# Identity products across a hand-over, and weight splits placed ahead of the folds

## The chip, the cores and the metric

The kernel runs on one core of a Trainium2 chip. The metric is the device time of one execution in microseconds (us); lower is better. A core has TensorE (PE in the profile, with its weight loads as PEld), VectorE (DVE), ScalarE (ACT), GpSimd (POOL) and SyncE (SP), which run their own instruction streams and meet on semaphores, and DMA queues that SP, ACT and POOL feed.

## The reference, cut to what matters

Four batches of 576 tokens, 512 features. Attention that keeps the top 32 scores of each row; a layer that sends each token to one of 8 experts; then a Fourier mixing layer with a two-layer network. All is float32.

```python
def _moe_ref(x, w_gate, w_local, w1, w2):          # experts
    ...
            h = np.maximum(x[b, s] @ w1[e], 0.0)
            out[b, s] = p[e] * (h @ w2[e])

def _moe2_ref(x, w_ch1, w_ch2):                    # mixer
    X = np.fft.fft(x, axis=1)
    X = np.fft.fft(X, axis=2)
    mixed = np.real(X).astype(np.float32)
    u = x + mixed
    mu = np.mean(u, axis=-1, keepdims=True)
    var = np.mean((u - mu) ** 2, axis=-1, keepdims=True)
    un = (u - mu) / np.sqrt(var + 1e-06)
    ch = np.maximum(un @ w_ch1, 0.0) @ w_ch2
    return (u + ch).astype(np.float32)
```

## The kernel before, in words

The program is a row of blocks: attention, routing, experts, mixer. In a block each engine has its own stream; at the end of a block all engines meet, and none starts the next block before the last has come.

**Early blocks.** Seven blocks of 128 tokens (NA = 7) go through their expert while attention and routing still run. Their hidden values and results live in the two buffers `stage[0]` and `stage[1]` (the `h`, `xT` and `y` of `early_buffers`). The last early result is scattered to the arrays `y_d` and `r_d` by POOL at the head of the experts' block (`early_scatter`, L264), and each of its two transfers adds to the semaphore `s_yo` of the early part. So far only POOL waits for that semaphore, at the very end of the experts' block.

**experts (L1080 on).** Fifteen blocks of 128 tokens. For each, PE multiplies the gathered tokens by `w1` (`hidden`, L1195: 32 float32 products of 128 columns, two records in the trace for each), turns the next block's tokens (L1183) and multiplies the hidden values by `w2`, split into a high and a low part (`output`, L1208 to L1210). ACT makes the high part (L1236), DVE the low part (L1252). SP's stream `load` decides block by block whether new weights have to be loaded: when the expert is the one already there it only raises the weight semaphore (L1167), otherwise it issues the DMA and that raises it. PE's `hidden` and ACT's split of `w2` wait for these semaphores, of the first block too. POOL gathers tokens (L1277) and scatters results (L1293).

**mixer (L1306 on).** For each batch: `fold` on DVE (L1715 to L1722) makes even and odd parts of the rows that SP (`xa`) and ACT (`xb`) have loaded; PE's `sequence` (L1478, five groups of three products) transforms along the tokens, ACT copies each group out (`u_out`, L1580), PE's `channels` (L1492, L1495) transforms along the features, ACT copies (`p_out`, L1589), DVE adds and takes moments (`low_high`, `add_a`, `moments`), ACT takes the square root (`spread`, L1596), DVE normalises (L1763), PE turns the tiles (`turn`, L1505), ACT copies them out (L1611). The network then runs in passes: PE's `hidden` and `output` (L1462 to L1464), with the following batch's transforms put in between. The network's weights come in 16 chunks of 512 KB through the two `stage` buffers; `split_w` on ACT (L1617) makes the high part of a chunk, `split_w` on DVE (L1768) the low part, and the load of chunk c (`load_w`, L1402) waits until chunk c - 2 has been split. All orders are written out by hand: an engine does its steps in the order of the code, so a step that waits holds back all that stands behind it.

In the mixer before, ACT does the first four `split_w` between `u_out` and `p_out`, and DVE does its first two behind the folds of the first batch and the other two behind those of the second.

Of the kernel before, what the change touches and what calls it, by code (L numbers as in the profile page):

```python
# [13 lines left out]
ACT = mybir.ActivationFunctionType  # L14
# [8 lines left out]
P = 128  # L23
# [13 lines left out]
NA = 7  # L37
# [1042 lines left out]
def experts(nc, env):  # L1080
# [5 lines left out]
    with ExitStack() as ctx:  # L1086
# [21 lines left out]
        ps_x = pb("ps_bx", [P, NC, P])  # L1108
# [12 lines left out]
        def used_blocks(eng):  # L1121
            return eng.value_load(env["blk_e"][0:1, NBLK + 2:NBLK + 3], min_val=0, max_val=NBLK)

        def blocks(eng, used, body):

            with eng.Fori(0, (SURE - 2) // 2) as i:
                for c in range(2):
                    body(i, c)
            for j in range((SURE - 2) // 2 * 2, SURE):
                body(j // 2, j % 2)  # L1130

            def rest(j):
                if j < NBLK:
                    with eng.If(used > j):
                        body(j // 2, j % 2)
                        rest(j + 1)

            rest(SURE)
# [12 lines left out]
        @block.sync  # L1151
        def _(sp):
            def expert(j):
                at = bass.ds(j + 2, 1) if not isinstance(j, int) else slice(j + 2, j + 3)
                return sp.value_load(env["blk_e"][0:1, at], min_val=0, max_val=E - 1)

            def load(i, c):
                j = 2 * i + c
                e, before = expert(j), expert(j - 2)

                def renew(load_w, s):

                    wait_apart(sp, s[c], 16 * i + 16, s_sp)
                    with sp.If(e != before):
                        load_w(sp, env, e, (NA + c) % 2, s[c])
                    with sp.Else():
                        sp.sem_inc(s[c], 16)  # L1167

                wait_apart(sp, s_h1, 2 * j + 2, s_sp)
                renew(load_w1, s_w1)  # L1170
                wait_apart(sp, s_w2lo, NQ * j + NQ, s_sp)
                renew(load_w2, s_w2)

            blocks(sp, used_blocks(sp), load)

        @block.tensor
        def _(pe):
            def turn(i, c, n):

                pe.wait_ge(s_x[c], 16 * (i + n // 2) + 16)  # L1180
                pe.wait_ge(s_xT, 2 * i + n + 1)
                for k in range(NC):
                    mm = pe.transpose(ps_x[:, k, :], x[c][:, k * P:(k + 1) * P], ident[:, :])  # L1183
                mm.then_inc(s_t, 1)

            def hidden(i, c):
                j = 2 * i + c
                pe.wait_ge(s_w1[c], 16 * i + 32)
                pe.wait_ge(s_xT, j + 2)
                for half in range(2):  # L1190
                    pe.wait_ge(s_hlo, 2 * j + half + 1)
                    for m in range(NF // 2):
                        f0 = (half * NF // 2 + m) * P
                        for k in range(NC):
                            mm = pe.matmul(ps_h[half][:, m, :], w1[c][:, k, f0:f0 + P], xT[c][:, k, :],  # L1195
                                           start=(k == 0), stop=(k == NC - 1))
                    mm.then_inc(s_h1, 1)

            def output(i, c):
                j = 2 * i + c  # L1200
                pe.wait_ge(s_yv, j + 1)
                for m in range(NF):
                    if m % (NF // 2) == 0:
                        pe.wait_ge(s_hlo, 2 * j + m // (NF // 2) + 3)
                    if m % (NF // NQ) == 0:
                        pe.wait_ge(s_w2lo, NQ * j + m // (NF // NQ) + 1 + 2 * NQ)
                    first, last = m == 0, m == NF - 1
                    pe.matmul(ps_y[c][:, :], h_hi[c][:, m, :], w2_hi[:, m, :], start=first, stop=False)  # L1208
                    pe.matmul(ps_y[c][:, :], h_hi[c][:, m, :], w2_lo[:, m, :], start=False, stop=False)
                    mm = pe.matmul(ps_y[c][:, :], h_lo[c][:, m, :], w2_hi[:, m, :], start=False, stop=last)  # L1210
                mm.then_inc(s_y, 1)

            for s, n in ((s_t, 2), (s_h1, 4), (s_y, 2)):
                pe.sem_inc(s, n)
            turn(0, 0, 0)
            used = used_blocks(pe)

            def body(i, c):
                hidden(i, c)
                if_used(pe, used, i, c + 1, lambda: turn(i, 1 - c, c + 1))  # L1220
                output(i, c)

            blocks(pe, used, body)

        @block.scalar
        def _(act):
# [81 lines left out]
def mixer(nc, env, w_ch, out):  # L1308
# [9 lines left out]
    NU = 5  # L1318
# [6 lines left out]
    with ExitStack() as ctx:  # L1325
        def sb(name, shape, dt=F32):
            return ctx.enter_context(nc.sbuf_tensor(name, shape, dt))
# [12 lines left out]
        p_sb = [sb(f"p_sb{n}", [P, HC + 1]) for n in range(2)]  # L1340
        lo = [sb(f"lo{n}", [P, HC + 1]) for n in range(2)]
        hi = [sb(f"hi{n}", [P, HC + 1]) for n in range(2)]
        stats = [sb(f"stats{w}", [P, 6]) for w in range(2)]
        mv = [[sb(f"mv{n}_{w}", [P, 2]) for w in range(2)] for n in range(2)]
        sd = [[sb(f"sd{n}_{w}", [P, 1]) for w in range(2)] for n in range(2)]
# [35 lines left out]
        def _(sp):  # L1381
            def load_a(n):
                r0, rows = rows_of(n)
                sp.dma_start(xa[n % RING][0:rows, :], env["y_d"][r0:r0 + rows, :]).then_inc(s_in[n % RING], 16)
# [12 lines left out]
                    load_b(n)  # L1397

            def load_w(c):
                if c >= 2:  # L1400
                    sp.wait_ge(s_wlo, c - 1)
                sp.dma_start(stage[c % 2][:, :], w_ch[c, :, :]).then_inc(s_stage[c % 2], 16)  # L1402

            def store_a(n):
# [16 lines left out]
                    r0 = (G * g + n) * P  # L1421
                    sp.dma_start(u[n][:, :], src[r0:r0 + P, :]).then_inc(s_ul[n], 16)

            for n in range(3):
                load_a(n)
            for c in range(2):
                load_w(c)
            for n in range(3, 6):
                load_a(n)
            for c in range(2, 6):  # L1430
                load_w(c)
# [28 lines left out]
        def _(pe):  # L1460
            def three(out_, hi1, lo1, hi2, lo2, first, last):
                pe.matmul(out_, hi1, hi2, start=first, stop=False)  # L1462
                pe.matmul(out_, hi1, lo2, start=False, stop=False)  # L1463
                return pe.matmul(out_, lo1, hi2, start=False, stop=last)  # L1464

            def sequence(b, m):

                part, tab = (ee, env["c_seq"]) if m < 3 else (oo, env["s_seq"])
                c0 = P * m if m < 3 else P * (m - 3)
                w = 1 if m == 2 else P  # L1470
                if m < 2:
                    pe.wait_ge(s_te, 6 * b)
                else:
                    pe.wait_ge(s_us, NU * b + m - 1)
                for k in range(3):
                    if m == 0:
                        pe.wait_ge(s_fold, 3 * b + k + 1)
                    mm = pe.matmul((ps_u, ps_t)[m % 2][0:w, 0:N1], part[b % 2][k][0:ROWS[k], c0:c0 + w],  # L1478
                                   tab[0:ROWS[k], k, :], start=(k == 0), stop=(k == 2))
                mm.then_inc(s_u, 1)  # L1480
# [70 lines left out]
                mm.then_inc(s_y, 1)  # L1551

            pe.wait_ge(env["s_tab"], 80)
            for m in range(NU):
                sequence(0, m)
            for n in range(3):
# [17 lines left out]
        def _(act):  # L1574
            def u_out(b, m):
                act.wait_ge(s_u, NU * b + m + 1)
                if b >= 1:
                    act.wait_ge(s_pq, 3 * b)
                w = 1 if m == 2 else P
                act.activation(us[m][0:w, :], (ps_u, ps_t)[m % 2][0:w, 0:N1], ACT.Copy).then_inc(s_us, 1)  # L1580
# [32 lines left out]
            def split_w(c):  # L1613
                act.wait_ge(s_stage[c % 2], 16 * (c // 2) + 16)
                if c >= NF:
                    act.wait_ge(s_y, NF * LAST_FIRST + c - NF + 1)
                act.activation(w_hi[:, c % NF, :], stage[c % 2][:, :], ACT.Copy).then_inc(s_whi, 1)  # L1617
# [44 lines left out]
            for n in range(6):  # L1662
                r0, rows = rows_of(n)
                act.dma_start(xb[n][0:rows, :], env["r_d"][r0:r0 + rows, :]).then_inc(s_in[n], 16)
            for m in range(3):
                u_out(0, m)
            split_w(0)
            u_out(0, 3)
            split_w(1)
            u_out(0, 4)  # L1670
            split_w(2)
            p_out(0)
            p_out(1)
            split_w(3)
            for w in range(2):
                spread(0, w)
            p_out(2)
# [25 lines left out]
        def _(dve):  # L1703
# [62 lines left out]
            def split_w(c):  # L1766
                dve.wait_ge(s_whi, c + 1)
                dve.tensor_tensor(w_lo[:, c % NF, :], stage[c % 2][:, :], w_hi[:, c % NF, :].bitcast(F32),  # L1768
                                  ALU.subtract).then_inc(s_wlo, 1)
# [23 lines left out]
            def between(q, f):  # L1793
# [22 lines left out]
                elif f == 5:  # L1816
# [3 lines left out]
                    normalise(n + 2, 0)  # L1820
                    normalise(n + 2, 1)

            for n in range(3):
                fold(n)
            split_w(0)
            split_w(1)
            for n in range(3, 6):
                fold(n)
            split_w(2)
            low_high(0)  # L1830
            add_a(0)
            moments(0, 0)
            low_high(1)
            split_w(3)
            moments(0, 1)
            add_a(1)
            normalise(0, 0)
# [190 lines left out]
```

## Time and profile before

| | us |
|---|---|
| median of 3 runs (1490.88 to 1491.41) | 1491.35 |
| the profiled execution's own time | 1492.38 |
| its span, first to last instruction | 1490.5 |
| PE busy in the span | 1378.8 |
| DVE busy | 1044.3 |
| POOL busy | 612.2 |
| ACT busy | 594.2 |

The profile is one execution. Times in it run from the span's start. A float32 product stands in it as two records. The granted clock is TensorE's, as a share of full speed: 1.00 is 2.4 GHz and 0.50 is 1.2 GHz, and a value between them is a mean over a stretch.

### The profile page before, as it was taken

The numbers are of one execution on the slowest core, as the hardware profiler recorded it, in microseconds if no ns is written. First come the engines' busy times: TensorE is split into PE (matmuls) and PEld (weight loads), VectorE is DVE, ScalarE is ACT, GpSimd is POOL, SyncE is SP. The second block draws the span as 40 slices with busy tenths as digits, with TensorE's granted clock in tenths as the row PEclk, the third lists the DMA queues.
The fourth block names the chain that finished last, engine by engine and source line by source line (L and its number), as shares of the span: only waits on it lengthen the run. The fifth ranks groups of instructions, "written<-read, shape, count | busy, mean of one in ns | idle before, by whom it ended". The sixth has DMA issues, their size and how long they took to land. (4 is left out here: it accounts for less than half of the span.)

```text
span 1490.5 us, 23027 instructions
## 1 busy us (share of the span) xinstructions
PE 1378.8 (93%) x7966; PEld 1128.1 (76%) x7966; DVE 1044.3 (70%) x2151; ACT 594.2 (40%) x1593; POOL 612.2 (41%) x491
## 2 busy tenths in 40 slices
PE   6889998999879999999989999967999999999998
PEld 4777777777657666777769999835877899999997
DVE  7999999999989999999965554446652522422221
ACT  4546555545426565556424444314222211311211
POOL 3666666666746767776414343302220200000000
PEclk9989898979879999999999999957999999999999
DMA  3101110001153434423354763543321211311111
GB/s 117 33 26 34 34 34 21 22 26 33 65 186 126 168 111 146 158 96 127 133 205 159 272 252 142 195 139 116 116 70 45 74 44 44 127 43 43 43 43 64
DMA packets 78131, 146.52 MB, mean 98 GB/s; under 512 B 27505, under 2 KB 27634, under 8 KB 78018
## 3 DMA queue, kind: packets, MB, share of 16 engines
q1 hardware_dynamic: 54170, 78.85, 16.1%
q10 hardware_dynamic: 14920, 39.23, 7.4%
q0 software_dynamic: 8928, 27.00, 5.0%
q8 instruction: 62, 1.02, 0.3%
q14 instruction: 51, 0.42, 0.1%
HBM read 116.74 MB, written 30.42 MB: 99 GB/s over the span
## 5 line engine op out<-in xcount | busy, mean ns | idle before, releaser
L674 POOL TENSOR_SCALAR keep<-s_sb,top 128x576 f32<-128x576 f32 x142 | 245.0, 1725 | 218.4 <-DVE top L701 218.2
L701 DVE MAX8 top<-w_sb 128x8 f32<-128x576 f32 x432 | 305.4, 747 | 0.0
L486 PEld LDWEIGHTS ps_o<-v_sb,eT 128*128 128x128 f32 (+1 forms) x1440 | 192.7, 196 | 61.0 <-issue 48.7
L1781 DVE SCALAR_TENSOR_TENSOR h_lo<-ps_ch,h_hi 128x384 fp32r<-128x384 f32 x96 | 53.5, 557 | 241.7 <-ACT h_hi L1632 241.6
L486 PE MATMUL ps_o<-v_sb,eT 128*128 128x74 f32 (+3 forms) x1440 | 218.6, 291 | 0.0
L703 DVE MATCH_REPLACE8 w_sb<-top,w_sb 128x576 f32<-128x576 f32 x288 | 211.8, 743 | 0.0
L678 POOL TENSOR_TENSOR e_sb<-e_sb,keep 128x576 f32<-128x576 f32 x142 | 200.3, 1411 | 27.2 <-ACT e_sb L590 6.0
L1632 ACT ACTIVATE h_hi<-ps_ch 128x384 fp32r<-128x384 f32 x96 | 47.2, 491 | 286.1 <-PE ps_ch L1464 286.1
L458 PE MATMUL ps_t<-ident,e_sb 128*128 128x128 f32 x576 | 101.3, 302 | 60.7 <-POOL e_sb L678 50.4
L1462 PE MATMUL ps_ch<-un_hi,w_hi 128*128 128x384 f32 x384 | 132.0, 344 | 1.6 <-DVE un_lo L1775 1.6
L579 ACT ACTIVATE eT<-ps_t 128x512 f32<-128x512 f32 x144 | 86.1, 598 | 110.3 <-PE ps_t L458 97.2
L1464 PE MATMUL ps_ch<-un_hi,w_lo 128*128 128x384 f32 x384 | 130.0, 339 | 0.0
L1463 PE MATMUL ps_ch<-un_lo,w_hi 128*128 128x384 f32 x384 | 129.5, 337 | 0.0
L440 PE MATMUL ps_s<-k_sb,q_sb 64*128 64x288 f32 x512 | 120.3, 501 | 7.0 <-DMA k_sb<-in_k 4.6
L458 PEld LDWEIGHTS ps_t<-ident,e_sb 128*128 128x128 f32 x576 | 64.9, 149 | 76.8 <-POOL e_sb L678 57.7
L599 ACT ACTIVATE s_sb<-ps_s 128x288 f32<-128x288 f32 x288 | 104.8, 406 | 40.2 <-PE ps_s L440 39.6
L590 ACT ACTIVATE e_sb<-s_sb,nmax 128x576 f32<-128x576 f32 x144 | 111.9, 777 | 13.5 <-ACT nmax L585 0.4
L1462 PE MATMUL ps_cy<-w_hi,h_hi 128*128 128x512 f32 x288 | 114.2, 396 | 0.0
L1464 PE MATMUL ps_cy<-w_hi,h_lo 128*128 128x512 f32 x288 | 113.3, 394 | 0.0
L1195 PEld LDWEIGHTS ps_h<-bxT,w 128*128 128x128 f32 x960 | 111.0, 194 | 2.9 <-issue 1.9
L1463 PE MATMUL ps_cy<-w_lo,h_hi 128*128 128x512 f32 x288 | 113.1, 393 | 0.0
L701 DVE MAX8 top<-s_sb 128x8 f32<-128x576 f32 x144 | 101.4, 743 | 16.6 <-ACT s_sb L599 16.6
(315 smaller groups left out, 2418.4 us busy)
## 6 DMA issues: line engine op xcount, KB each, us to landing
w<-in_w ACTq DMA_DIRECT2D x18, 2048.0 KB, 8.4
w<-in_w SPq DMA_DIRECT2D x14, 2048.0 KB
stage<-in_w_ch SPq DMA_DIRECT2D x16, 512.0 KB, 3.3
q_sb<-in_q SPq DMA_DIRECT2D x16, 288.0 KB, 2.8
vT<-in_vt SPq DMA_DIRECT2D x16, 288.0 KB, 3.1
x_d<-rows SPq DMA_DIRECT2D x18, 256.0 KB, 5.2
u<-u_d SPq DMA_DIRECT2D x18, 256.0 KB, 2.9
x_d<-u POOLq DMA_DIRECT2D x18, 256.0 KB, 2.6
```

What stands on the lines that cost most here:

```text
L440: return pe.matmul(ps_s[k % 2][:, 0:SH], lhsT, k_sb[b][rows, h * SH:(h + 1) * SH], start=True, stop=True)
L458: mm = pe.transpose(ps_t[:, c * P:(c + 1) * P], e_sb[k % NE][:, c * P:(c + 1) * P], ident[:, :])
L486: mm = pe.matmul(ps_o[k % 2][:, lo:hi], eT[k % NT_][0:n, c, :], v_sb[b][0:n, c, lo:hi], start=(c == 0), stop=(c == KC))
L590: act.activation(e_sb[k % NE][:, :], s_sb[k % NS][:, :], ACT.Exp, bias=nmax[:, k % NE:k % NE + 1], scale=SCALE).then_inc(s_exp, 1)
L674: pool.tensor_scalar(keep[t % 2][:, :], s_sb[t % NS][:, :], top[t % NS][:, TOPK - 1:TOPK], None, ALU.is_ge).then_inc(s_keep, 1)
L678: pool.tensor_tensor(e_sb[t % NE][:, :], e_sb[t % NE][:, :], keep[t % 2][:, :], ALU.mult).then_inc(s_mask, 1)
L701: dve.max(eight, src).then_inc(s_top, 1)
L703: dve.match_replace(out=w_sb[k % 2][:, :], in_to_replace=eight, in_values=src, imm_value=-BIG).then_inc(s_top, 1)
L1195: mm = pe.matmul(ps_h[half][:, m, :], w1[c][:, k, f0:f0 + P], xT[c][:, k, :], start=(k == 0), stop=(k == NC - 1))
L1462: pe.matmul(out_, hi1, hi2, start=first, stop=False)
L1463: pe.matmul(out_, hi1, lo2, start=False, stop=False)
L1464: return pe.matmul(out_, lo1, hi2, start=False, stop=last)
```

## The change

- SP, experts: before its loop SP waits until all early scatters have landed (`s_yo` at 32 * NA), and then issues the loads of weight chunks 0 and 1 into the two `stage` buffers. The mixer's SP stream no longer issues them, and loads the first six tiles `xa` in one go.
- PE, experts: behind the last block, 36 products of the identity with itself.
- PE, mixer: `keep_clock`, 24 identity products before the first `sequence`, and 6 each before the waits for the second and third fold.
- ACT, mixer: behind its six DMA issues a square root of one column (`warm`), then `split_w` 0 to 3, then the five `u_out` and the rest as it was.
- DVE, mixer: `split_w` 0 and 1, the folds of the first batch, `split_w` 2 and 3, the folds of the second batch, then the rest without `split_w`.

```diff
@@ experts, sync
-            blocks(sp, used_blocks(sp), load)
+            used = used_blocks(sp)
+            sp.wait_ge(env["early"]["s_yo"], 32 * NA)
+            for c in range(2):
+                sp.dma_start(env["stage"][c][:, :], env["w_ch"][c, :, :]).then_inc(env["s_stage"][c], 16)
+            blocks(sp, used, load)
@@ experts, tensor
             blocks(pe, used, body)
+            for _ in range(36):
+                pe.matmul(ps_x[:, 0, :], ident[:, :], ident[:, :], start=True, stop=True)
@@ mixer
+        warm = sb("warm", [P, 1])
@@ mixer, sync
             def load_w(c):
-                if c >= 2:
-                    sp.wait_ge(s_wlo, c - 1)
+                sp.wait_ge(s_wlo, c - 1)
@@
-            for n in range(3):
-                load_a(n)
-            for c in range(2):
-                load_w(c)
-            for n in range(3, 6):
+            for n in range(6):
                 load_a(n)
             for c in range(2, 6):
                 load_w(c)
@@ mixer, tensor
+            def keep_clock(count):
+
+                for _ in range(count):
+                    pe.matmul(ps_h[0][:, 0:P], ident[:, :], ident[:, :], start=True, stop=True)
+
@@ sequence
                 for k in range(3):
                     if m == 0:
+                        if b == 0 and k > 0:
+                            keep_clock(6)
                         pe.wait_ge(s_fold, 3 * b + k + 1)
@@
             pe.wait_ge(env["s_tab"], 80)
+            keep_clock(24)
             for m in range(NU):
                 sequence(0, m)
@@ mixer, scalar
-            for m in range(3):
+            act.activation(warm[:, :], env["cst"][:, C_EPS:C_EPS + 1], ACT.Sqrt)
+            for c in range(4):
+                split_w(c)
+            for m in range(NU):
                 u_out(0, m)
-            split_w(0)
-            u_out(0, 3)
-            split_w(1)
-            u_out(0, 4)
-            split_w(2)
             p_out(0)
             p_out(1)
-            split_w(3)
@@ mixer, vector
+            split_w(0)
+            split_w(1)
             for n in range(3):
                 fold(n)
-            split_w(0)
-            split_w(1)
+            split_w(2)
+            split_w(3)
             for n in range(3, 6):
                 fold(n)
-            split_w(2)
             low_high(0)
             add_a(0)
             moments(0, 0)
             low_high(1)
-            split_w(3)
             moments(0, 1)
```

## Rows read from the trace of the kernel before

**Rows 1.** Busy time by stage, all engines: PE, PEld, DVE, ACT, POOL, granted clock, DMA share, GB/s.

```profile
784.00:966.00 182.00, 182.00 (x1283) 168.35 (x1282) 93.24 (x98) 76.06 (x97) 72.61 (x66) 1.00 0.57 209
...
979.60:1023.50 43.90, 33.41 (x84) 17.09 (x85) 29.19 (x75) 13.68 (x28) 8.78 (x12) 0.58 0.36 124
```

**Rows 2.** Timeline at the head of the experts' block.

```profile
766.69 0.63 PE L1183 MATMUL ps_bx<-ident,x 128*128 128x128 f32 x4 [2.02 <-ACTq L1242]
...
768.91 1.01 POOL L264 DMA_INDIRECT r_d<-stage,early_sidx  x1 [0.30 <-issue]
768.96 9.04 PE L1195 MATMUL ps_h<-bxT,w 128*128 128x128 f32 x64 [1.64 <-DMA w<-in_w]
769.71 3.90 ACT L1236 ACTIVATE w_hi<-w 128x1024 fp32r<-128x1024 f32 x4 [1.76 <-SPq L1167]
```

**Rows 3.** POOL's DMA queue, 772 to 774, then 776 to 778 (40 slices of 0.05).

```profile
q0 software_dynamic: 145, 0.46, 63.1%
...
GB/s 0 82 0 0 82 0 0 82 0 0 82 0 0 82 0 0 0 0 0 0 0 0 0 0 0 0 0 0 0 0 0 0 0 0 0 0 0 0 0 0
...
q0 software_dynamic: 7, 0.02, 2.6%
```

**Rows 4.** Timeline: an expert's first product, then the hand-over.

```profile
940.52 7.31 PE L1195 MATMUL ps_h<-bxT,w 128*128 128x128 f32 x64
...
965.98 0.39 PE L1210 MATMUL ps_y<-w_hi,bh_lo 128*128 128x512 f32 x1
...
973.59 2.92 ACTq L1664 DMA_DIRECT2D xb<-r_d  x6
975.00 0.83 SPq L1402 DMA_DIRECT2D stage<-in_w_ch  x2
...
977.45 0.69 DVE L1715 TENSOR_TENSOR un<-xa,xb 128x512 f32<-128x512 f32 x1 [10.06 <-DMA xb<-r_d]
...
979.64 1.30 PE L1478 MATMUL ps_u<-c_seq,ee 128*128 128x289 f32 x2 [13.27 <-DVE oo L1722]
```

**Rows 5.** Granted clock (third number from the end) in short stretches, experts and mixer.

```profile
770.00:772.00 2.00, 2.00 (x12) 2.00 (x11) 1.20 (x2) 2.00 (x3) 1.18 (x2) 0.50 0.93 309
772.00:774.00 2.00, 2.00 (x15) 2.00 (x15) 2.00 (x3) 1.61 (x2) 0.92 (x1) 0.74 1.00 366
...
1004.00:1006.00 2.00, 2.00 (x7) 1.11 (x5) 1.94 (x6) 0.39 (x1) 0.63 (x2) 0.72 0.22 59
1010.00:1012.00 2.00, 0.00 (x0) 0.00 (x0) 1.96 (x6) 0.72 (x3) 1.23 (x2) 0.99 0.69 131
1012.00:1014.00 2.00, 1.37 (x7) 1.37 (x8) 1.90 (x6) 0.00 (x0) 1.00 (x1) 0.50 0.94 357
...
1028.00:1030.00 2.00, 2.00 (x7) 0.93 (x5) 1.37 (x2) 1.16 (x2) 0.00 (x0) 0.74 0.00 0
```

**Rows 6.** Timeline of the mixer's head.

```profile
984.71 3.56 PE L1478 MATMUL ps_ft<-c_seq,ee 128*128 128x289 f32 x6
...
1001.95 2.07 PE L1495 MATMUL ps_pq<-s_ch,us 128*128 128x255 f32 x4
...
1004.48 0.42 DVE L1731 TENSOR_TENSOR lo<-p_sb,ps_pq 128x255 f32<-128x255 f32 x1
...
1008.57 1.28 ACT L1596 ACT_TABLE_LOAD   x1
1008.59 1.23 DVE L1768 TENSOR_TENSOR w_lo<-stage,w_hi 128x1024 fp32r<-128x1024 f32 x1 [0.19 <-ACT w_hi L1617]
1009.73 0.69 DVE L1753 BATCH_NORM_STATS2 stats<-xb 128x6 f32<-128x512 f32 x1
1009.87 0.29 ACT L1596 ACTIVATE sd<-mv,cst 128x1 f32<-128x1 f32 x1
```

**Rows 7.** Timeline: the network's first product and transforms at full clock.

```profile
1023.51 0.66 PE L1462 MATMUL ps_ch<-un_hi,w_hi 128*128 128x384 f32 x1 [1.61 <-DVE un_lo L1775]
...
1035.78 1.92 PE L1478 MATMUL ps_ft<-s_seq,oo 128*128 128x289 f32 x6
```

## The prediction

> **What bounds the kernel now.** I read the page first: PE is busy for 1378.8 of 1490.5 us, so time is won or lost where PE stands still or runs at half clock. Next I read the busy time by stage. [rows 1] show two kinds. In 784 to 966 (experts) PE is busy for 182.00 of 182.00 us at a granted clock of 1.00: nothing in there can absorb a delay, and whatever delays the first expert block delays the end by as much. In 979.6 to 1023.5 (the mixer's head) PE is busy for 33.4 of 43.9 us and the mean clock is 0.58: here the folds, the transforms at half speed and the chain through DVE set the pace. From 1023.5 on PE is nearly full again. So both places that the change touches are on the path that sets the end.
>
> The timeline at the head of the experts' block is read for what starts PE. [rows 2]: PE turns the first tokens at 766.69, then has nothing until 768.96, when `hidden` starts. ACT's split of `w2` starts at 769.71 and its idle time is ended by SP's L1167. This is the branch in which no weights are loaded and SP only raises the semaphore. PE's `hidden` waits for the same kind of signal. So a stream that looks idle, SP's, releases the whole stage, 2.3 us after the block's first work. In the same rows POOL issues the second transfer of the last early scatter at 768.91, so it is not even issued when SP today has passed that point.
>
> **Step 1, SP's new wait (the largest term).** SP now waits, ahead of its loop, until that scatter has landed. Queued behind the wait are the two `stage` loads and every weight semaphore of the loop; PE's `hidden` and ACT's and DVE's split of `w2` wait for these. When does it land? POOL's queue is busy with 145 packets in 772 to 774, and its last data packets run at about 776.7 [rows 3]. Three transfers of 80 packets share that queue, the two scatters and a gather behind them, so the scatters cannot be complete before about 774, and may be complete as late as 776.7. I take 776.7, because a transfer is complete only when its slowest part is, and both kinds of transfer have a part on the same late engine. Then come two issues, 0.83 us [rows 4], and the path from block entry to the first release, at most 2.3 us, of which some is spent ahead of the wait: I take 2.1 (bounds 1.5 and 2.3). First release: 776.7 + 0.8 + 2.1 = 779.6 against 768.9 now, **+10.8 us**. Low bound: 774.0 + 0.8 + 1.5 = 776.3, +7.4. The `w2` release comes 0.7 behind as now, and its split takes less than PE's 9.0 us of `hidden`, so it adds nothing. Nothing hides the delay: PE has no idle time behind it until 966 [rows 1].
>
> **Step 2, PE's clock at that restart.** PE will now have stood still from 767.3 to 779.7. Today the clock is at 0.50 in all of 770 to 772 and back at about 773.0 (0.74 in 772 to 774) [rows 5], some 3.4 us at half speed. The other restart in the trace, at 1023.51, gets full clock at about 1029.0 ([rows 5], 0.74 in 1028 to 1030), 5.5 us. I take 5.1 us from the start. The extra 1.7 us at half speed cost **+0.8 us**; bounds 0, and +5.6 if all 64 records ran at half speed (14.6 us at twice the 0.114 us of [rows 4], against 9.04).
>
> **Step 3, the identity products.** At full clock 64 records take 7.31 us [rows 4]. The 36 products are 72 records: 8.1 us from 966.2 to 974.3. The last to come to the meeting of the engines is today POOL, and the mixer starts at 973.59 [rows 4]. Now it is PE, at about 974.6 with its drain: the mixer opens **1.2 us** later. The 24 products then run from about 974.9 to 980.3.
>
> **Step 4, splits ahead of the folds.** The fold starts today at 977.45, when `xb` lands [rows 4]. Afterwards: opening 974.8, ACT's six issues 2.9 us, table load 1.28 and square root 0.29 [rows 6] to 979.2, then two high parts (four take 3.90 [rows 2], about 1.0 each) and two low parts of 1.23 [rows 6] in a pipeline: high parts done at 980.3 and 981.25, low parts at 981.5 and 982.6. The first fold starts at 982.6, **5.2 us** later than now (1.2 of it is step 3). The loads hoisted out of SP's stream save nothing here: the tiles have landed by then anyway. PE gets the first fold at 984.8 (2.2 behind, as now), having run out of identity products at 980.3. That is 4.5 us of idle. In [rows 5] the clock was 0.99 in 1010 to 1012 with PE idle throughout, and 0.50 in all of 1012 to 1014, where PE worked again: an idle time of little over 2 us was followed by the fall. So I expect it to fall here too, before the first transform.
>
> [...]
>
> **Step 5, the transforms.** First product of `sequence` from 984.8 at half clock 1.2 us, six identity products 2.6 us, second product 1.2, and so on. With full clock again 3.4 to 6.8 us after the restart (the rows of step 2), the first group ends at 991.0 to 992.6; I take 991.8, against 984.7 now [rows 6]. From there I win: a group of six records takes 1.92 us at full clock [rows 7] against 3.56 [rows 6]. The four groups that now take 984.7 to 998.3, 13.6 us, take 7.3; `channels` of the first tile 2.8 in place of 5.2. Its end: 991.8 + 7.3 + 0.5 + 2.8 = 1002.4 against 1004.0 now. Splits 2 and 3 and the second batch's folds end on DVE at about 997, ahead of that: hidden. If they had no cover they would cost 2.4 + 5.9.
>
> **Step 6, DVE's chain.** `low_high(0)` starts at 1002.9 (1004.48 now). The second `channels` ends at 1005.1, `low_high(1)` at 1006.3, and the moments that now start at 1009.73 [rows 6], behind a 1.23 us split and with ACT's table load beside it, start at about 1006.0: **-3.7 us**, the 1.2 of step 3 included. From there DVE is the bound until 1021 and is not changed. PE stands still between its turns as now, so the network's first product starts at half clock as now. Chunks 4 and up load earlier, which nothing waits for.
>
> **Sum.** +10.8 + 0.8 - 3.7 = +7.9 us. Against the profiled execution, 1492.38, that is 1500.3; against the median, which is 1.03 lower, 1499.2.
>
> The Trainium skill (ScalarE: Activation LUTs, What ACT_TABLE_LOAD costs) adds a drain of 1.38 us to the load's 1.28. By it the first fold would come 1.4 us later still. The trace disagrees: the load starts at 1008.57 and the square root behind it at 1009.87, 1.30 later [rows 6].
>
> **Rivals.**
> 1. *The clock holds through the hand-over* (other side). If the 4.5 us gap does not drop it, the first group is bound by the folds alone and ends at 989.4 (-2.4 more), and if it also holds through DVE's chain the network's 5.5 us at half clock and the turns give 3.2. The mixer then wins 9.3 and the total is +10.8 + 0.8 - 9.3 = +2.3: 1493.7, within 0.2%. It decides at a mixer gain of 8.6 us. Against it: the falls after short idle time in [rows 5]. 0.12.
> 2. *The clock stays low through the transforms.* Now it stays at 0.50 from 979 to 1005 although PE is busy without a gap from 984.7 [rows 5, 6]; these products do not lift it quickly. If the identity products between them don't either, the first group ends at 993.9 (+9.1), the groups take as long as now, and only the split and table load (-1.9) come off: +10.8 + 0.8 + 7.2 = +18.8, 1510.2. For it: that stretch. Against: identity products of the same form as `hidden`, which brought the clock back in 3.4 us [rows 5]. 0.10.
> 3. *The wait does not bite*: the early scatter has landed when SP comes. Then only the mixer counts: 1487.7, faster by 0.25%. Against it: the transfer is issued at 768.91 [rows 2]. 0.07.
> 4. *A drain beside the moved table load*: 1500.6. Against it: 1.30 us from load to square root [rows 6]. 0.05.
>
> **How the numbers follow.** The forecast has 0.66. Its own range is 1494.5 to 1501.5 (step 1 at 8, clock 0, mixer -4.9; or 10.8, 1.7, -2.3). The range for 8 in 10 reaches down to rival 1 and leaves out rivals 2 and 3: 1493.5 to 1503. A measurement of this kernel tells a change from none at about 0.2%, 3.0 us. Slower by more: the forecast, rivals 2 and 4, less the forecast's low edge: 0.80. Within: rival 1: 0.12. Faster: rival 3 and the edge of rival 1: 0.08.
>
> **What the profile would show.** Step 1: the first L1195 at 779 to 780, its idle time ended by a semaphore of SP's, and PE full behind it up to about 977. Step 2: the granted clock at 0.50 for 4 to 7 us there. Step 3: identity products last ahead of the meeting. Step 4: the first fold some 9 us after the mixer opens, DVE's L1768 ahead of it, and a PE gap of over 4 us. Step 5: `ps_ft` groups of 1.9 us. Step 6: the network's first product 3 to 5 us earlier after the experts' last product than now (57.5 us). The prediction is wrong if L1195 starts near 769, or if the clock never falls behind 980.

## The result and the profile after

| | before | changed |
|---|---|---|
| median of 20 runs, us | 1491.94 (1489.41 to 1504.61) | 1499.93 (1496.93 to 1507.83) |
| span of the profiled execution | 1490.5 | 1499.6 |

The ratio of the undisturbed runs is 1.0043 (95% interval 1.0024 to 1.0061): slower by 3.6 to 9.1 us, with 6.4 us in the middle; the medians are 8.0 us apart. The sum of the prediction was +7.9 us. The runs of one kernel scatter by over 10 us. One source shows in the traces: the head of the experts' block lies between 765.1 and 774.5 us in the fourteen traces of this study, although nothing ahead of it differs. Traces are therefore compared from that head on.

The busy time by stage of the changed kernel, with the columns of [rows 1], shows the experts' block as full as before, a head of the mixer at a higher mean clock (0.77 for 0.58), and the places where the clock moves.

```profile
795.00:977.00 182.00, 182.00 (x1283) 168.29 (x1282) 93.19 (x98) 76.17 (x97) 72.56 (x66) 1.00 0.57 209
995.00:1034.00 39.00, 27.14 (x109) 17.37 (x110) 30.58 (x80) 11.03 (x26) 8.36 (x12) 0.77 0.29 103
782.00:784.00 2.00, 2.00 (x11) 2.00 (x11) 2.00 (x3) 1.82 (x2) 0.00 (x0) 0.50 0.00 0
784.00:786.00 2.00, 2.00 (x19) 2.00 (x18) 1.64 (x2) 0.52 (x1) 0.00 (x0) 0.92 0.00 0
994.00:996.00 2.00, 0.00 (x0) 0.00 (x0) 2.00 (x3) 0.08 (x1) 0.00 (x0) 0.99 1.02 354
996.00:998.00 2.00, 0.38 (x1) 0.41 (x2) 2.00 (x8) 0.00 (x0) 0.00 (x0) 0.50 0.98 356
1002.00:1004.00 2.00, 2.00 (x14) 1.74 (x13) 2.00 (x3) 0.00 (x0) 0.00 (x0) 0.80 0.16 35
```

The timeline of the changed kernel at the head of the experts' block answers to [rows 2].

```profile
767.83 0.63 PE L1187 MATMUL ps_bx<-ident,x 128*128 128x128 f32 x4 [2.02 <-ACTq L1248]
...
770.04 1.01 POOL L264 DMA_INDIRECT r_d<-stage,early_sidx  x1 [0.30 <-issue]
...
776.14 0.81 SPq L1177 DMA_DIRECT2D stage<-in_w_ch  x2
779.16 7.07 PE L1199 MATMUL ps_h<-bxT,w 128*128 128x128 f32 x39 [10.70 <-SPq L1167]
779.92 3.90 ACT L1242 ACTIVATE w_hi<-w 128x1024 fp32r<-128x1024 f32 x4 [10.83 <-SPq L1167]
```

The reader is to see four things in a row: the scatter issued at 770.04, SP's two loads only at 776.14, PE's first expert product at 779.16, and its idle time of 10.70 us ended by SP's L1167, the increment that means "these weights are there". What SP itself waited for stands in the view of its queue's waits (us in total, times, longest):

```profile
SPq L1177 <- DMA r_d<-stage,early_sidx: 8.2, 1, 8.2
```

This is the second transfer of the last early scatter. From the turn of the first tokens to the first product it is now 11.3 us in place of 2.3.

The timeline of the hand-over and of the mixer's head answers to [rows 4] and [rows 6].

```profile
977.18 0.39 PE L1214 MATMUL ps_y<-w_hi,bh_lo 128*128 128x512 f32 x1
977.43 1.94 PE L1229 MATMUL ps_bx<-ident 128*128 128x128 f32 x15
...
980.81 6.63 PE L1229 MATMUL ps_bx<-ident 128*128 128x128 f32 x57 [1.44 <-issue]
981.08 0.97 POOL L1299 DMA_INDIRECT r_d<-y,at_y  x1 [0.30 <-issue]
...
987.82 2.84 ACTq L1674 DMA_DIRECT2D xb<-r_d  x6
987.86 5.60 PE L1471 MATMUL ps_ch<-ident 128*128 128x128 f32 x48 [0.42 <-PEq L1086]
990.69 1.28 ACT L1675 ACT_TABLE_LOAD   x1 [17.96 <-issue]
991.98 0.20 ACT L1675 ACTIVATE warm<-cst 128x1 f32<-128x1 f32 x1
992.09 1.99 ACT L1627 ACTIVATE w_hi<-stage 128x1024 fp32r<-128x1024 f32 x2
993.17 2.36 DVE L1775 TENSOR_TENSOR w_lo<-stage,w_hi 128x1024 fp32r<-128x1024 f32 x2 [14.59 <-ACT w_hi L1627]
...
995.44 0.68 DVE L1722 TENSOR_TENSOR un<-xa,xb 128x512 f32<-128x512 f32 x1
...
997.62 1.30 PE L1487 MATMUL ps_u<-c_seq,ee 128*128 128x289 f32 x2 [4.17 <-DVE oo L1729]
...
1004.62 1.92 PE L1487 MATMUL ps_ft<-c_seq,ee 128*128 128x289 f32 x6
...
1012.39 1.14 PE L1501 MATMUL ps_pq<-c_ch,us 128*128 128x257 f32 x4 [0.50 <-ACT us L1590]
...
1015.67 0.42 DVE L1738 TENSOR_TENSOR lo<-p_sb,ps_pq 128x255 f32<-128x255 f32 x1 [6.16 <-ACT p_sb L1599]
...
1018.88 0.68 DVE L1760 BATCH_NORM_STATS2 stats<-xb 128x6 f32<-128x512 f32 x1
```

The mixer opens at 987.8, 10.6 us behind the start of the last expert product (7.6 before). PE has stood only 0.42 us before its first `keep_clock` product: PE itself is now the last to come. The 72 records have a hole of 1.44 us behind the fifteenth. The first fold comes 7.6 us behind the opening (3.9 before), and PE has been idle for 4.17 us when it gets it; the clock falls in that gap (0.99 in 994 to 996, 0.50 in 996 to 998). It is back within 1002 to 1004, and the groups behind that take 1.9 us.

Where the 8.0 us of the trace went, in us, read from the start times of the two timelines:

| stretch | before | changed |
|---|---|---|
| turn of the first tokens to first expert product | 2.3 | 11.3 |
| to the last expert product | 197.0 | 198.0 |
| to the mixer's opening | 7.6 | 10.6 |
| to the first fold | 3.9 | 7.6 |
| to the second group of transforms | 7.3 | 9.2 |
| to the first `channels` | 14.1 | 7.8 |
| to the first `low_high` | 5.7 | 3.3 |
| to the moments of `xb` of the first tile | 5.3 | 3.2 |
| to the network's first product | 13.8 | 14.9 |
| to the last product | 462.4 | 461.1 |
| sum | 719.2 | 727.1 |

### The profile page after: what moved, and what is told of

The parts are those of the page before. It is cut to its first block and busy times, and to the rows that moved or that the text cites. A ratio compares the mean times of both kernels' runs of the same rounds, so it can differ in the third digit from the quotient of the medians.

```text
span 1499.6 us, 23316 instructions
## 1 busy us (share of the span) xinstructions
PE 1386.8 (92%) x8110; PEld 1142.6 (76%) x8110; DVE 1044.9 (70%) x2151; ACT 595.2 (40%) x1594; POOL 610.5 (41%) x491
## 3 DMA queue, kind: packets, MB, share of 16 engines
q8 instruction: 63, 1.03, 0.3%
## 5 line engine op out<-in xcount | busy, mean ns | idle before, releaser
L1199 PE MATMUL ps_h<-bxT,w 128*128 128x128 f32 x960 | 112.1, 279 | 10.7 <-SPq L1167 10.7
## 6 DMA issues: line engine op xcount, KB each, us to landing
w<-in_w SPq DMA_DIRECT2D x14, 2048.0 KB, 11.4
```

## Experiments

All were timed against the kernel before on the same chip; ratios are to it. "Late loads" means the wait and the two loads placed behind SP's loop. The last column of the table further down sums all from the first expert product on.

**e1, without the hoist.**

```diff
-            used = used_blocks(sp)
-            sp.wait_ge(env["early"]["s_yo"], 32 * NA)
-            for c in range(2):
-                sp.dma_start(env["stage"][c][:, :], ...)
-            blocks(sp, used, load)
+            blocks(sp, used_blocks(sp), load)
```

with the two `load_w` back in the mixer.

> The changed kernel with SP's wait and its two stage loads taken out of the experts' block and back in the mixer; all else as changed. My theory (the wait costs 10 us at the experts' head, the mixer wins 2): the first L1199-like product is back 2.3 us behind the block's first work, the experts' 10.2 us come off, but the two chunks now land some 8 us behind their issue, 3 to 4 us after ACT could split them: about 1492, within 0.2% of the kernel before. Rival (the mixer's new order is what costs): stays at about 1499.

Measured: median 1496.29 against 1492.97, ratio 1.0027 (1.0005 to 1.0049). The experts' start is back at 2.3 us, as expected, but the total is higher than I said: the chunks cost more in the mixer than the 3 to 4 us that I allowed. The timeline of this run:

```profile
984.45 0.83 SPq L1405 DMA_DIRECT2D stage<-in_w_ch  x2
...
991.11 1.06 ACT L1628 ACTIVATE w_hi<-stage 128x1024 fp32r<-128x1024 f32 x1 [3.65 <-DMA stage<-in_w_ch]
...
993.10 1.06 ACT L1628 ACTIVATE w_hi<-stage 128x1024 fp32r<-128x1024 f32 x1 [0.93 <-DMA stage<-in_w_ch]
994.18 1.23 DVE L1776 TENSOR_TENSOR w_lo<-stage,w_hi 128x1024 fp32r<-128x1024 f32 x1 [0.76 <-ACT w_hi L1628]
995.33 0.68 DVE L1723 TENSOR_TENSOR un<-xa,xb 128x512 f32<-128x512 f32 x1
```

ACT waits 3.65 and again 0.93 us for chunks that SP issues only behind the first three tiles, and the first fold comes 12.2 us behind the opening. So the splits ahead of the folds need the loads early; they are two parts of one change. My sum of 1492 had left out the 3.0 us of the meeting, which this run still has.

**e2, the hoist alone** (added to the kernel before).

> The kernel before with SP's wait and the two hoisted loads alone. My theory: first hidden product 10 to 11 us behind the turn of the first tokens in place of 2.3, clock back up 4 to 7 us later, the end 9 to 11 us later: 1501 to 1502. Rival (the delay is caught up in the experts' block, or the earlier loads give it back in the mixer): within 3 us of the kernel before.

Measured: median 1501.48 against 1492.97, ratio 1.0057 (1.0027 to 1.0087). 11.4 us from turn to first product, 198.1 to the last. The timeline shows the same wait in a kernel whose mixer is the old one:

```profile
773.56 0.81 SPq L1177 DMA_DIRECT2D stage<-in_w_ch  x2
776.59 3.77 PE L1199 MATMUL ps_h<-bxT,w 128*128 128x128 f32 x16 [10.36 <-SPq L1167]
```

SP waits 8.2 us for the early scatter here too, and its two issues take 0.8. The wait with its two loads is shown to cost some 9 us without any other part of the change, and nothing gives them back. No run has the loads without the wait, so their share is read from these rows.

**e3, late loads** (all else as changed).

```diff
-            used = used_blocks(sp)
+            blocks(sp, used_blocks(sp), load)
             sp.wait_ge(env["early"]["s_yo"], 32 * NA)
             for c in range(2):
                 sp.dma_start(env["stage"][c][:, :], ...)
-            blocks(sp, used, load)
```

> The changed kernel with the wait and the two loads behind SP's loop over the expert blocks in place of ahead of it; all else as changed. My theory: the experts start as before, the mixer keeps its 2 us: 1489 to 1490, 10 us under the changed kernel. Rival (the loads themselves disturb the experts' block, wherever they stand): above 1495.

Measured: median 1489.28, ratio 0.9967 (0.9939 to 0.9995). From the first expert product on it takes 715.7 us, as the changed kernel does (715.8); the 9 us ahead of that product are gone, so that it takes 718.0 us from the turn of the first tokens, against 727.1. Behind the loop the wait and the loads cost nothing that shows; ahead of it they cost 9 us.

**e4, late loads and no products at the end of the experts' block** (the loop of 36 taken out).

> As the third run, without the 36 identity products at the end of the experts' block. My theory: they hold back the meeting of the engines by 3 us and the clock falls before the first transform with or without them; the mixer opens 3 us earlier and the end comes 2 to 3 us earlier than in the third run: 1486 to 1488. Rival (they hold the clock through the meeting): the 24 products then run at half clock, 10.7 us in place of 5.4, past the first fold, and the end is the same or up to 3 us later.

Measured: median 1486.90, ratio 0.9950 (0.9927 to 0.9974), 2.4 us under e3, with which it was timed side by side. The traces differ by more, 711.1 us against 715.7: 3.0 us of it are the earlier opening, the rest lies in the transforms and behind the network's first product. The timeline:

```profile
974.75 2.86 ACTq L1671 DMA_DIRECT2D xb<-r_d  x6
974.79 7.53 PE L1468 MATMUL ps_ch<-ident 128*128 128x128 f32 x48 [7.25 <-PEq L1086]
...
984.58 0.72 PE L1484 MATMUL ps_u<-c_seq,ee 128*128 128x289 f32 x2 [2.26 <-DVE oo L1726]
```

The opening is 7.6 us behind the last expert product again. The rival is half right: the 24 products do start at half clock and take 7.5 us in place of 5.6, but they end 2.26 us ahead of the first fold's result, so they delay nothing. My theory was wrong on one point: the clock was still at 1.00 when that result came (the first two transform records took 0.72 us, 1.30 in the changed kernel) and fell at 985.7, to come back at 989.0. The expectation for e5 has this fall too early, ahead of the first fold.

**e5, no identity product at all** (e4 without `keep_clock(24)` and the two `keep_clock(6)`).

> The changed kernel with the wait and the two loads behind SP's loop over the expert blocks, and with no identity product at all; the splits and the square root stand as changed. In the fourth run (no 36, but 24 and 6 + 6) the clock fell ahead of the first fold and rose 4.5 us after it. My theory: the products between the folds bring the clock back; without them the transforms run at half clock as in the kernel before (first group to channels 14 us in place of 8), channels 5 us in place of 3: the end 5 to 8 us later than in the fourth run, 1492 to 1495. Rival (the gain of the fourth run comes from the moved splits and square root alone): within 2 us of the fourth run.

Measured: median 1495.63 against 1492.81, ratio 1.0025 (1.0005 to 1.0044). The timeline of PE:

```profile
995.08 3.55 PE L1482 MATMUL ps_ft<-c_seq,ee 128*128 128x289 f32 x6
998.56 3.13 PE L1482 MATMUL ps_u<-c_seq,ee 128*1 128x289 f32 x6
...
1005.11 3.55 PE L1482 MATMUL ps_u<-s_seq,oo 128*128 128x289 f32 x6
1009.16 2.08 PE L1496 MATMUL ps_pq<-c_ch,us 128*128 128x257 f32 x4 [0.50 <-ACT us L1584]
```

Each group of full width takes 3.5 us, as in [rows 6]: PE is busy with one gap of 0.50 us and stays at half clock. The splits and the square root placed ahead, without the products, make the kernel slower than it was: they delay the first fold by 3.8 us and PE's transforms do not repay it. In this order the whole gain of the mixer hangs on the clock. Not tried is the reverse, identity products alone in the order of the kernel before, and neither was the earlier square root by itself.

**e6, the folds first on DVE** (e4 with `split_w` 0 to 3 between the folds of the first and the second batch).

> The fourth run (late loads, no 36 products, 24 and 6 + 6 kept) with DVE's four splits between the folds of the first and the second batch, none ahead of the first fold. My theory: the 4 us between the mixer's opening and the first fold come back (3.9 in place of 7.6), but the 24 products, at half clock after the meeting, take up to 10.7 us less what the clock's return gives, and hold back the first transform to 982 to 985: the first group ends 1 to 3 us earlier than in the fourth run, the end 0 to 3 us earlier, 1484 to 1487. Rival (the splits ahead of the folds were hidden all along): no difference, 1487.

Measured: median 1495.16, ratio 1.0015 (0.9992 to 1.0037). Neither theory. The fold comes 4.1 us behind the opening as I said, the clock is up again at 976.1, and then the gain is lost:

```profile
984.10 8.08 SPq L1405 DMA_DIRECT2D stage<-in_w_ch  x4
987.33 1.06 ACT L1624 ACTIVATE w_hi<-stage 128x1024 fp32r<-128x1024 f32 x1 [8.87 <-DMA stage<-in_w_ch]
989.51 1.06 ACT L1624 ACTIVATE w_hi<-stage 128x1024 fp32r<-128x1024 f32 x1 [1.12 <-DMA stage<-in_w_ch]
990.47 0.40 ACT L1587 ACTIVATE us<-ps_u 128x289 f32<-128x289 f32 x1
...
990.92 3.14 PE L1484 MATMUL ps_u<-c_seq,ee 128*1 128x289 f32 x6 [5.13 <-ACT us L1587]
```

ACT's third split stands ahead of all its copies. It waits for a chunk that SP loads only behind DVE's first split, which now comes after the folds. The copies wait behind it, PE waits 5.13 us for a copy, and the clock falls (3.14 us for a group of one row in place of 1.7). The half clock then costs 3.7 us more up to the network's first product (25.1 in place of 21.4). I had moved one engine's steps and not traced who waits for them.

**e7, the same with 24 products at the end of the experts' block.**

> As the sixth run, with 24 identity products at the end of the experts' block (the change has 36). My theory: they end about 7 us behind the last expert product, the hole of 1.4 us in them included, so that POOL's scatter still is the last to come and the mixer opens no later (7.6 us behind the last product); the clock holds through the meeting and the 24 products of the mixer, the transforms start at full clock, and the end comes 3 to 6 us earlier than in the fourth run: 1481 to 1484. Rival (a longer end of the experts' block delays the meeting whatever its length): opening 2 us later and no gain over the sixth run.

Measured: median 1495.47, ratio 1.0023 (1.0005 to 1.0041). It has the wait of e6 (18.2 us from the second group to `channels`), so it says nothing on the end. What it does say: the clock held at 1.00 from the experts to 987.2, and the opening came 8.7 us behind the last product, 1.1 later than without.

**e8, late loads in the kernel before.**

> The kernel before with the wait and the two loads behind SP's loop over the expert blocks, and nothing else. My theory: nothing in the kernel before waits for chunks 0 and 1, whose split stands behind the transforms, so the hoist alone is worth nothing: within 1 us of the kernel before. Rival (1 MB less beside the first tiles lets them land earlier): first fold up to 1 us nearer to the opening, and the end as much earlier.

Measured: median 1491.14 against 1492.81, ratio 0.9982 (0.9962 to 1.0003), no difference that this tells apart. The trace has no gain either: 717.3 us from the first expert product on, against 716.9. The early loads are worth something only to an order that splits early (e1 against e3).

**e9, both engines moved** (late loads, 18 products at the experts' end):

```diff
 # scalar
-            for c in range(4):
+            for c in range(2):
                 split_w(c)
             for m in range(NU):
                 u_out(0, m)
+                if m in (2, 3):
+                    split_w(m)
 # vector
-            split_w(0)
-            split_w(1)
             for n in range(3):
                 fold(n)
-            split_w(2)
-            split_w(3)
+            split_w(0)
+            split_w(1)
             for n in range(3, 6):
                 fold(n)
+            split_w(2)
+            split_w(3)
```

> Late loads; folds ahead of the splits on DVE as in the sixth run, and ACT's splits 2 and 3 moved too, behind its third and fourth copy of a transform; 18 identity products at the end of the experts' block, 24 and 6 + 6 kept. My theory (in the sixth and seventh runs ACT's third split, which waits for a chunk that is loaded only behind DVE's first split, held back the copies of the transforms and PE with them for 5 us): no such wait, opening 7.6 us behind the last expert product, first fold 3.9 behind it, clock at 1.00 from the experts to the channels, first network product 40 to 42 us behind the opening in place of 49.9 before and 45.1 in the fourth run: 1482 to 1484. Rival (folds ahead of the splits cannot win, DVE's total ahead of the first low_high sets the time): 45 us and 1487.

Measured: median 1482.76 against 1492.78, ratio 0.9919 (0.9889 to 0.9949). 40.8 us from the opening to the network's first product (45.2 in e4, 49.9 before). One part was wrong: the clock did dip, to 0.50 from 980.0 to 983.4, so the 18 products did not carry it through the meeting.

**e10, the same without those 18.**

> As the ninth run, without the products at the end of the experts' block. My theory: the clock falls in the meeting, the mixer's 24 products bring it back 4 to 7 us behind the opening and the last of them end 1 to 2 us past the first fold: the end 0.5 to 2 us later than in the ninth run. Rival (the products in the experts' block are what keeps the gain): 5 us or more later, the transforms at half clock.

Measured: median 1483.45, ratio 0.9935 (0.9909 to 0.9962); 0.7 us above e9, within the scatter. No gain of the products ahead of the meeting shows; from the opening to the network's first product the traces have 40.8 us with them and 41.2 without.

**e11, only the 6 + 6** (e4 without `keep_clock(24)`).

> The fourth run (late loads, splits ahead of the folds, no 36) without the 24 products too: only the 6 + 6 between the folds are left. My theory: the clock is lost before the first fold with or without the 24; the 6 + 6 bring it back in the first group, as in the changed kernel: the end 0 to 1.5 us later than in the fourth run, 1487 to 1488. Rival (the 24 are needed): the transforms run at half clock as in the fifth run, 1495.

Measured: median 1488.05, ratio 0.9981 (0.9950 to 1.0011). From the first expert product on 711.3 us, e4 711.1. With e5 at 720.6, the traces have twelve products between the folds carry the whole 9 us that the identity products bring in this order. The medians, of runs that were not timed side by side, give 7.6 of 8.7 us. The busy time by stage shows what they do, first e5 and then e11, with the clock third from the end:

```profile
995.00:1010.00 15.00, 14.50 (x27) 6.18 (x27) 6.89 (x19) 2.05 (x5) 0.00 (x0) 0.50 0.22 70
988.00:1000.00 12.00, 11.50 (x41) 5.88 (x41) 6.29 (x21) 2.44 (x6) 0.00 (x0) 1.00 0.28 85
```

**e12, e9 with products where PE waits for DVE's chain.**

```diff
             for n in range(3):
+                for _ in range((10, 12, 4)[n]):
+                    pe.matmul(ps_y[0][:, 0:P], ident[:, :], ident[:, :], start=True, stop=True)
                 for w in range(2):
                     turn(n, w)
+            for _ in range(6):
+                pe.matmul(ps_y[0][:, 0:P], ident[:, :], ident[:, :], start=True, stop=True)
```

> As the ninth run, with 10, 12 and 4 more identity products ahead of the three tiles' turns and 6 ahead of the network's first product, where PE waits for DVE's chain. My theory: the clock stays at 1.00 there, the network's first 3 to 7 us run at full clock: the end 1.5 to 3.5 us earlier than in the ninth run. Rival (the products end behind what they wait for, and the turns come later): no gain, or up to 1 us lost.

Measured: median 1482.14, ratio 0.9935 (0.9905 to 0.9965). The busy time by stage, first of e9 and then of this run, shows the clock (third from the end) held through the chain and into the network:

```profile
1001.00:1021.00 20.00, 11.28 (x51) 7.03 (x49) 16.29 (x42) 6.72 (x19) 8.36 (x12) 0.74 0.39 130
1021.00:1028.00 7.00, 7.00 (x24) 5.53 (x24) 2.99 (x5) 2.30 (x5) 0.00 (x0) 0.76 0.32 115
```

```profile
995.00:1015.30 20.30, 18.18 (x118) 13.52 (x117) 16.78 (x43) 6.71 (x19) 8.56 (x12) 1.00 0.37 125
1015.30:1022.00 6.70, 6.70 (x29) 4.94 (x30) 3.02 (x5) 2.75 (x6) 0.00 (x0) 1.00 0.47 155
```

The trace gains 1.3 us on e9 (705.1 against 706.4), the medians 0.6 us; the timing cannot tell them apart. e9 and e12 both beat the kernel before by some 10 us, and the changed one, by medians that were not timed side by side, by some 17.

Stretches of the traces in us: a, turn of the first tokens to first expert product; b, last expert product to opening; c, to the first fold; d, to the second group; e, to `channels`; f, to the network's first product; g, first expert product to last product.

| | a | b | c | d | e | f | g |
|---|---|---|---|---|---|---|---|
| before | 2.3 | 7.6 | 3.9 | 7.3 | 14.1 | 24.7 | 716.9 |
| changed | 11.3 | 10.6 | 7.6 | 9.2 | 7.8 | 21.4 | 715.8 |
| e1 | 2.3 | 10.3 | 12.2 | 8.3 | 7.8 | 21.4 | 719.5 |
| e2 | 11.4 | 7.6 | 4.0 | 7.2 | 14.1 | 24.9 | 718.4 |
| e3 | 2.3 | 10.7 | 7.7 | 9.0 | 7.8 | 21.4 | 715.7 |
| e4 | 2.3 | 7.6 | 7.6 | 8.3 | 7.8 | 21.4 | 711.1 |
| e5 | 2.3 | 7.6 | 7.7 | 7.2 | 14.1 | 25.1 | 720.6 |
| e6 | 2.3 | 7.6 | 4.1 | 7.7 | 17.6 | 25.1 | 720.8 |
| e7 | 2.3 | 8.7 | 3.6 | 6.8 | 18.2 | 25.1 | 721.5 |
| e8 | 2.3 | 7.6 | 4.0 | 7.2 | 14.1 | 26.3 | 717.3 |
| e9 | 2.3 | 7.6 | 4.9 | 6.7 | 7.8 | 21.4 | 706.4 |
| e10 | 2.3 | 7.6 | 4.1 | 7.8 | 7.8 | 21.5 | 708.0 |
| e11 | 2.3 | 7.6 | 7.8 | 8.7 | 7.8 | 21.0 | 711.3 |
| e12 | 2.3 | 7.6 | 5.5 | 6.7 | 7.8 | 20.8 | 705.1 |

## Why the prediction was right, step by step

**Step 1** was right in mechanism and 1.8 us too large: +9.0 measured (e2 alone: +9.1) against +10.8; the terms as written, 779.6 less 768.9, give 10.7. I took the landing at the last packets of POOL's queue, 776.7; SP was released at 776.1 in a trace whose experts' head lies 1.1 us later, so at 775.0 on the old clock. The packets behind that are most likely those of the gather, which is issued last; the views do not tell the three transfers apart. The path from there to the first product took 3.0 us, against my 2.9.

**Step 2**: +1.0 measured, +0.8 forecast; 0.50 until about 784.2.

**Step 3** was the term that I undersized: 3.0 us, not 1.2. The count of products and their 0.11 us were right, the hole of 1.44 us was not in my sum. Rival sums had no such case either.

**Step 4**: 7.6 us from opening to fold against 7.8 forecast, and the fall of the clock in PE's gap as described. **Step 5**: 9.2 us to the second group (forecast 9.2) and 7.8 to `channels` (7.8). The upper end of its "3.4 to 6.8 us after the restart" stands in none of the rows of step 2, which give 3.4 and 5.5; the restarts of the runs took 3.3 (e9) to 5.2 us (changed, both at 779.16 and at 997.62). **Step 6**: 3.3 and 3.2 us as forecast (3.3 and 3.1), but "from there DVE is not changed" failed by 1.1 us: 14.9 in place of 13.8. The timeline of DVE and POOL in the changed kernel:

```profile
1018.55 0.41 DVE L1739 TENSOR_TENSOR hi<-p_sb,ps_ch 128x255 f32<-128x255 f32 x1
...
1020.37 0.74 POOL L1881 TENSOR_TENSOR xb<-xb,hi 128x255 f32<-128x255 f32 x1
1020.38 1.02 DVE L1746 TENSOR_TENSOR xa<-xa,lo 128x255 f32<-128x255 f32 x1
1021.05 0.93 POOL L1882 TENSOR_TENSOR xb<-xb,lo 128x255 f32<-128x255 f32 x1
1021.32 0.94 DVE L1748 TENSOR_TENSOR xa<-xa,hi 128x255 f32<-128x255 f32 x1
```

Additions of the same shape take 0.41 alone and 1.02 and 0.94 here, where POOL's additions for the same tile (1020.37 to 1022.0) now run beside them. With DVE's split gone from between them, the two engines meet. The other traces bear this out. Where POOL's two additions for this tile end before DVE's begin (before, e2, e8; 1010.51 and 0.71 us against 1011.17 in the kernel before), DVE's take 0.41 us each and the stretch is 13.6 to 13.8 us. Where the two pairs start together (changed, e1, e3, e4, e9, e10), DVE's take 1.02 or 1.03 and 0.94 and the stretch is 14.9 to 15.0. The other five traces lie between, with 13.9 to 14.5. No run changes POOL's additions alone.

From the last expert product to the network's first one the changed kernel takes 56.6 us, before 57.5: it won 0.9 us in place of 3.7, because of the 1.8 us more of step 3 and the 1.1 us of step 6. Step 1 was too large by 1.8 us, and the stretch behind the network's first product was 1.2 us shorter, which I had not counted; e3, with the same mixer code, has 462.2 us there, against 462.4 before and 461.1 in the changed kernel, so this does not show as a gain of the change. That the errors cancel, +8.0 in the traces against +7.9, is luck. What each step says of the order of events is borne out by its own rows, but for the hole of step 3 and the additions of step 6.

**Rivals.** The first (the clock holds) fell in the changed kernel at step 4's gap. With an order that leaves no such gap and 24 products ahead of the meeting it came true (e7: 1.00 from the experts to 987.2), but there another wait took the gain. With 18 products the clock fell in the meeting (e9) or right behind it (e12, at 975.3); e12 then held it through DVE's chain. The second (identity products don't bring the clock back) is excluded by e5 against e11. The third (the wait does not bite) is excluded by e2 and by the 8.2 us that SP waited. The fourth, a drain at the moved table load, is excluded by the trace: load at 990.69, next ACT operation at 991.98, 1.29 us later. The Trainium skill (ScalarE: Activation LUTs, What ACT_TABLE_LOAD costs) gives 1.38 us more; no run here shows it.

## What to carry to other kernels

A stream that only issues loads may also be the one that releases compute: before a wait is put at its head, list every semaphore that the stream raises behind it, also on the branch that loads nothing. The same wait with its two loads cost 9 us at one end of SP's loop and nothing at the other.

Steps moved on one engine have to be followed through the others. e6 won 3.5 us at the fold and lost 10 in a wait that ran SP, ACT, PE. Identity products pay where PE's own work leaves the clock at 1.2 GHz: here twelve of them between the folds were enough. Those ahead of an all-engine meeting gained nothing that was measured; 36 of them delayed it by 3.0 us and 24 by 1.1.

## What the runs showed of the hardware

- PE can be busy almost without a break and stay at half clock: in e5, for 14.5 of the 15 us from 995 to 1010, at 0.50, in groups of 3.55 us. Twelve identity products among the first three products were enough for the clock to rise and then stay up through the same transforms (e11: 1.00 from 988 to 1000).
- The idle time ahead of a fall of the clock was not one number: 2.0 us in e9 (from 978.0), 2.3 in the kernel before (from 1009.7), 2.5 in the changed one (from 993.5), 4.0 in e6 (from 985.8) and 4.3 in e11 (from 964.9).
- Behind the end of a loop nest with branches PE ran 15 records and then stood for 1.44 us, with "issue" as the only cause. In the five other runs with products there the hole was again behind the fifteenth record (1.17 us in e1, 1.58 in e3, 1.53 in e7, 0.84 in e9 and 0.99 in e12). Its cause is open. A wait for instructions is possible, but the packets of the instruction queue do not show it: the changed kernel has one at 978.1, 1.3 us ahead of the hole, and the kernel before (966.8) and e4 (967.9) have the same one behind their last expert product, where PE has nothing to run.
- DVE additions of 128x255 took 0.41 or 0.42 us alone and 0.94 to 1.03 us beside POOL's. Overlap alone is not enough: the addition at 1016.74 in the changed kernel began 0.1 us ahead of POOL's and took 0.42, and it was POOL's that took longer (0.90 us, against 0.74 for the same one at 1020.37).
